# Attention and two MLPs in one kernel: the pooled v through DRAM, the pooled k on VectorE, the root in PSUM, and a new order up to the second tile

## The chip, the cores and the metric

The kernel runs on one core of one Trainium2 chip. The metric is the device time of one execution, in microseconds; it is the median of several runs. Before the change it is 1004.99 us (three runs, 1004.07 to 1005.27).

## The reference

q, k and v are [4, 8, 576, 64] (batch, head, position, channel). The output of the attention is the sum of two attentions, and goes through two MLPs.

```python
q_d, k_d, v_d = [t.reshape(B, H, 144, 4, D).mean(axis=3) for t in (q, k, v)]
out_up = np.repeat(softmax(scale * q_d @ k_d.T) @ v_d, 4, axis=2)      # pooled: 144 x 144 a head
scores = np.where(abs(i - j) < 4, scale * q @ k.T, -1e9)               # local: a band of 7
x = out_up + softmax(scores) @ v                                       # -> [2304, 512]
xn = x / sqrt(mean(x * x, -1) + 1e-6) * rms_g
y = (silu(xn @ w_gate) * (xn @ w_val)) @ w_out                         # 512 -> 1536 -> 512
out = (s * relu(y @ w_in) ** 2 + b) @ w2_out                           # 512 -> 2048 -> 512
```

Both softmaxes subtract the row's maximum and divide by the sum (+ 1e-9). Everything is float32.

## The kernel before

**Tiles.** A row of the MLPs is one position of one batch with its eight heads side by side, 512 channels. A partition holds four neighbouring positions (f = 0 to 3), so a tile is 128 partitions times 4 = 512 rows, and 2304 rows are four whole tiles and one of 256 rows. Tile 0 enters the first MLP in two halves of 256 rows (chunks (0, 1) and (2, 3) of f).

**Pooled attention.** Per batch, four neighbouring rows of q, k and v are summed. q (`pool_q`, L1512) is summed on VectorE in two additions of 128x1152 and 128x576 elements (L1516, L1518); k (`pool_k`, L1127) on GpSimd in three additions of 128x576 (L1133, L1135, L1137). v is needed with 72 partitions, as it is an operand of the last product with the sum over keys in two halves of 72. It is loaded that way (`load_rawv`, L992, two halves a batch into three buffers) and summed in additions of 72x1024 and 72x512: batches 1 and 2 on VectorE (`pool_v`, L1534), batch 3 on GpSimd (`pool_v3`, L1141). Batch 0 has functions of its own (`pool_q0`, `pool_k0`, `pool_v0`) that the change leaves.
TensorE turns the sums (L1835), and for each of 32 heads n computes the scores (L1847), turns the exponentials of head n - 2 (L1858) and multiplies those of head n - 3 with `dv` (L1884). VectorE takes each head's minimum (`least`, L1559), ScalarE its exponentials (`exponents`, L1252) and evacuations (`keep_pooled`, `keep_turned`). `finish_pooled` (L1551) writes `co`, ScalarE stores it to `c_scr` in DRAM (`store_co`), and SyncE loads it back tile by tile as `ct`.

**Local attention.** For each tile, sixteen half heads n: GpSimd multiplies windows of q and k (`qk_mult`, L549, 128x896 elements), VectorE sums (`qk_reduce`, L594); softmax on VectorE and ScalarE (`softmax_max`, `softmax_exp`, `softmax_norm`); then sixteen products of probabilities and windows of v, twelve on GpSimd (`pv_mult`, L563), four on ScalarE (`pv_taps`, L576), again summed on VectorE (L604, L586). The products have two buffers, `prod`, so GpSimd is at most two ahead of VectorE. `add_pooled` adds `ct`, ScalarE sums the squares, VectorE takes the inverse root (`inverse_root`, L673: an estimate from the bits, three Newton steps, each operation on 128x4 elements, each waited for by the next), ScalarE scales (`normalise`), TensorE transposes (L717).

**MLPs.** Numbers are split into a high and a low part and each product is three matrix products. Step s of the first MLP takes 128 of the 1536 hidden columns: `gate` and `val` (L774) with 24 products, `silu` (ScalarE), `hidden_mul` (VectorE, L830), `hidden_hi` (ScalarE), `hidden_lo` (VectorE, L836), and two steps later `out1` (L808 to L810) with 12. Steps 0 to 5 and 6 to 11 are the two halves of tile 0 (256 columns) over the first half of the hidden columns, steps 12 to 17 all of tile 0 (512 columns) over the second; tile 1 begins at step 18. The weights come in 18 pieces through four slots: SyncE loads (`load_piece`, L433), ScalarE makes the high part (`weight_hi`), VectorE or GpSimd the low one (`weight_lo`, L426); a slot is free for the next load once its low part is made.

**Order.** Each engine has its own queue and takes its instructions in the written order; waits are on semaphores and stand in that queue. SyncE issues nearly all loads in a written order, ScalarE the stores. On every engine the order of all this up to the second tile is written out by hand, call by call; later tiles follow tables (`QK_REST`, `PV_LATE` and others). On ScalarE, for one, the end of the second tile's attention stands as follows:

```python
            squares(act, 1, 0)      # L1425
            silu(act, 14)
            pv_taps(act, 1, 13, 0)
            pv_taps(act, 1, 13, 1)
            hidden_hi(act, 14)
            squares(act, 1, 1)
            silu(act, 15)
```

## Time and profile before

| what | value |
|---|---|
| median of the runs | 1004.99 us |
| the profiled execution's own time | 1007.7 us |
| its span, first to last instruction | 1005.6 us |
| TensorE busy | 962.9 us (96%) |
| VectorE, ScalarE, GpSimd busy | 543.8, 354.8, 407.2 us |
| read from and written to HBM | 66.17 and 10.62 MB |

Times in the rows are microseconds from the start of the span of the profiled execution. TensorE is PE, VectorE DVE, ScalarE ACT, GpSimd POOL, SyncE SP. "[a <-b]" behind a row is idle time of the engine before it and the instruction that ended it. An instruction's length includes the time in which it has begun and is held up.

### The profile page before, as it was taken

The numbers are of one execution on the slowest core, as the hardware profiler recorded it, in microseconds if no ns is written. First come the engines' busy times: TensorE is split into PE (matmuls) and PEld (weight loads), VectorE is DVE, ScalarE is ACT, GpSimd is POOL, SyncE is SP. The second block draws the span as 40 slices with busy tenths as digits, with TensorE's granted clock in tenths as the row PEclk, the third lists the DMA queues.
The fourth block names the chain that finished last, engine by engine and source line by source line (L and its number), as shares of the span: only waits on it lengthen the run. The fifth ranks groups of instructions, "written<-read, shape, count | busy, mean of one in ns | idle before, by whom it ended". The sixth has DMA issues, their size and how long they took to land.

```text
span 1005.6 us, 12924 instructions
## 1 busy us (share of the span) xinstructions
PE 962.9 (96%) x4864; PEld 767.7 (76%) x4864; DVE 543.8 (54%) x790; ACT 354.8 (35%) x816; POOL 407.2 (40%) x211
## 2 busy tenths in 40 slices
PE   5899879899999999999999999999999999999997
PEld 4666679766777777777777998888888888888886
...
GB/s 266 227 201 200 110 153 221 119 81 46 141 65 81 39 104 89 27 35 56 38 1 126 85 128 104 42 1 84 1 0 42 42 1 1 64 1 1 0 43 21
DMA packets 53549, 77.62 MB, mean 77 GB/s; under 512 B 6320, under 2 KB 37008, under 8 KB 52464
## 3 DMA queue, kind: packets, MB, share of 16 engines
...
HBM read 66.17 MB, written 10.62 MB: 76 GB/s over the span
## 4 chain that ended last, share of the span: by engine, by line
PE 77%; DVE 5%; POOL 4%; DMA 4%; SPq 3%; ACT 3%; issue 2%; ACTq 0%; DVEq 0%; POOLq 0%
PE bank L774 24%; PE bank L914 7%; PE bank L915 7%; PE bank L916 6%; PE bank L897 6%; PE bank L898 6%; PE bank L896 6%; PE bank L810 4%; PE bank L808 4%; PE bank L809 4%; POOL prod L549 3%; SPq L515 2%; ACT prod_a L576 1%; DMA rawv<-in_v_dram 1%; DMA ks<-in_k_dram 1%
## 5 line engine op out<-in xcount | busy, mean ns | idle before, releaser
L549 POOL TENSOR_TENSOR prod<-qs,ks 128x896 f32<-128x896 f32 x80 | 176.7, 2230 | 90.9 <-DVE sc L594 67.1
L563 POOL TENSOR_TENSOR prod<-sc,vs 128x896 f32<-128x896 f32 x72 | 136.7, 2000 | 47.6 <-DVE x L604 29.0
L935 DVE SCALAR_TENSOR_TENSOR r<-bank,r 128x512 f32<-128x512 f32 (+1 forms) x80 | 51.0, 638 | 181.1 <-ACT r L923 181.1
L898 PE MATMUL bank<-y_h,w2i_l 128*128 128x512 f32 (+1 forms) x320 | 117.7, 368 | 0.0
L923 ACT ACTIVATE r<-bank 128x512 f32<-128x512 f32 (+1 forms) x80 | 44.4, 555 | 182.0 <-PE bank L898 181.3
L830 DVE TENSOR_TENSOR bank<-bank,u 128x512 f32<-128x512 f32 (+1 forms) x66 | 39.5, 599 | 125.4 <-PE bank L774 124.5
L774 PE MATMUL bank<-x_h,wv_h 128*128 128x512 f32 (+1 forms) x264 | 100.9, 393 | 2.6 <-DVE h_l L836 2.6
L808 PE MATMUL bank<-h_h,wo_h 128*128 128x512 f32 (+1 forms) x264 | 103.0, 390 | 0.0
L594 DVE TENSOR_REDUCE sc<-prod 128x14 f32<-128x896 f32 x80 | 85.4, 1077 | 21.4 <-POOL prod L549 21.3
L810 PE MATMUL bank<-h_h,wo_l 128*128 128x512 f32 (+1 forms) x264 | 93.5, 354 | 0.0
L809 PE MATMUL bank<-h_l,wo_h 128*128 128x512 f32 (+1 forms) x264 | 92.8, 351 | 0.0
L774 PE MATMUL bank<-x_h,wg_h 128*128 128x512 f32 (+1 forms) x264 | 89.2, 359 | 2.6 <-ACT u L818 2.5
L774 PE MATMUL bank<-x_l,wv_h 128*128 128x512 f32 (+1 forms) x264 | 91.3, 357 | 0.0
L774 PE MATMUL bank<-x_l,wg_h 128*128 128x512 f32 (+1 forms) x264 | 88.2, 356 | 0.3 <-DVE x_l L752 0.3
L604 DVE TENSOR_REDUCE x<-prod 128x128 f32<-128x896 f32 x72 | 77.6, 1080 | 15.9 <-POOL prod L563 15.3
L914 PE MATMUL bank<-w2o_ha,g_h 128*128 128x512 f32 x216 | 84.3, 390 | 0.4 <-ACT y_st L844 0.4
L915 PE MATMUL bank<-w2o_la,g_h 128*128 128x512 f32 x216 | 84.2, 390 | 0.0
L916 PE MATMUL bank<-w2o_ha,g_l 128*128 128x512 f32 x216 | 84.0, 389 | 0.0
L929 ACT ACTIVATE g_h<-r 128x512 fp32r<-128x512 f32 (+1 forms) x80 | 47.1, 589 | 101.0 <-DVE r L937 101.0
L818 ACT ACTIVATE u<-bank 128x512 f32<-128x512 f32 (+1 forms) x66 | 34.3, 520 | 130.5 <-PE bank L774 129.4
L943 DVE TENSOR_TENSOR g_l<-r,g_h 128x512 fp32r<-128x512 f32 (+1 forms) x80 | 51.1, 639 | 52.5 <-ACT g_h L929 52.5
L824 ACT ACTIVATE h_h<-bank 128x512 fp32r<-128x512 f32 (+1 forms) x66 | 34.2, 519 | 110.7 <-DVE bank L830 110.7
...
## 6 DMA issues: line engine op xcount, KB each, us to landing
...
```

Source lines behind the costliest of these rows:

```text
L549: pool.tensor_tensor(dst, qv, kv, ALU.mult).then_inc(prod_ready, 1)
L563: pool.tensor_tensor(dst, pv, vv, ALU.mult).then_inc(prod_ready, 1)
L594: dve.tensor_reduce(sc[:, a % 2, n * 2 * BAND:(n + 1) * 2 * BAND], prod[:, at_ % 2, :].rearrange("p (s d) -> p s d", d=D), op=ALU.add, axi ...
L604: dve.tensor_reduce(x[:, 2 * half:2 * half + 2, h * D:(h + 1) * D], over(prod[:, at_ % 2, :], [[BAND * D, 2], [BAND, D], [1, BAND]]), op=A ...
L774: last = pe.matmul(o[:, 0:w], wt[:, m, kk, :], xs[:, kk, cols], start=i == 0, stop=i == 3 * DT - 1)
L808: pe.matmul(o, wo_h[:, m, cols], h_h[:, s % 3, 0:w], start=m == 0 and p != 1, stop=False)
L809: pe.matmul(o, wo_h[:, m, cols], h_l[:, s % 3, 0:w], start=False, stop=False)
L810: last = pe.matmul(o, wo_l[:, m, cols], h_h[:, s % 3, 0:w], start=False, stop=m == M1 - 1)
L898: last = pe.matmul(o, w2i_l[:, m, kk, :], y_h[t % 2][:, kk, 0:w], start=False, stop=kk == DT - 1)
L914: pe.matmul(o, g_h[:, r % 3, cols], wh[:, mh, :], start=m == 0, stop=False)
L915: pe.matmul(o, g_h[:, r % 3, cols], wl[:, mh, :], start=False, stop=False)
L916: last = pe.matmul(o, g_l[:, r % 3, cols], wh[:, mh, :], start=False, stop=m == M2 - 1)
```

## The change

- v of batches 1 to 3 is loaded as k and q are, in 128 partitions, but with nine neighbouring rows to a partition, one load a batch, each into a buffer of its own. `pool_v` sums it into `vd` with additions of 128x1152 and 128x576. ScalarE stores `vd` to a DRAM tensor `v_scr` (`store_vd`), and SyncE loads it from there in 72 partitions into `dv` (`load_dv`), waiting for the store and for the buffer. TensorE waits for that load.
- k of batches 1 to 3 is summed by two additions on VectorE, `pool_k(dve, b)`, no longer by three on GpSimd; nor does GpSimd sum v of batch 3.
- The inverse root has its mean, its product and a second copy of its estimate in a PSUM bank: bank 5 (`CTR`) for tile 0, bank 4 (`XT[0]`) for the others. The sums of squares are first brought there by a reduction.
- The low parts of the weights: GpSimd made pieces 0, 1, 2, 5, 7, 9, 11, 13 and 15; it now makes 0, 14 and 17, VectorE the others.
- The order on all queues up to the second tile is written anew.

The diff, with its order lists cut:

```diff
     c_scr = nc.dram_tensor("c_scr", [G, E], F32, kind="Internal").ap()
...
-        rawv += [place([at[0]], "rawv2", [P, H, FAC * D], F32)]
-        at[0] += QT * FAC * D * 4
+        rawv = [None, rawv[1], place(at, "rawv2", [P, QT, FAC * D], F32), rawv[2]]
...
         rawk0_loaded = [sem(f"rawk0_loaded{g}") for g in range(3)]
         rawv0_loaded = [sem(f"rawv0_loaded{g}") for g in range(2)]
         q0_pooled, k0_pooled, v0_pooled = sem("q0_pooled"), sem("k0_pooled"), sem("v0_pooled")
-        rawv_loaded = [sem(f"rawv_loaded{i}") for i in range(3)]
-        q_pooled, k_pooled, v_pooled, k_order = sem("q_pooled"), sem("k_pooled"), sem("v_pooled"), sem("k_order")
-        v3_pooled, v_order = sem("v3_pooled"), sem("v_order")
+        rawv_loaded = [sem(f"rawv_loaded{b}") for b in range(B)]
+        vd_stored, dv_loaded = sem("vd_stored"), [sem("dv_loaded0"), sem("dv_loaded1")]
+        k_order, q_pooled = sem("k_order"), sem("q_pooled")
...
-        def inverse_root(dve, a, c):
-
-            a_link(dve, dve.tensor_scalar(var[:, c], var[:, c] if a else sqs[:, c], 1.0 / E, 1e-6, ALU.mult, ALU.add))
-            dve.tensor_scalar_mul(halfv[:, c], var[:, c], -0.5)
-            a_link(dve, dve.tensor_scalar(rinv[:, c].bitcast(I32), var[:, c].bitcast(I32), -0.5, float(RSQRT_BITS), ALU.mult, ALU.add))
+        def inverse_root(dve, scratch):
+
+            var, newt, root = [scratch[:, i * FAC:(i + 1) * FAC] for i in range(3)]
+            a_link(dve, dve.tensor_scalar(var, var, 1.0 / E, 1e-6, ALU.mult, ALU.add))
+            dve.tensor_scalar_mul(halfv[:, :], var, -0.5)
+            dve.tensor_scalar(rinv[:, :].bitcast(I32), var.bitcast(I32), -0.5, float(RSQRT_BITS), ALU.mult, ALU.add)
+            a_link(dve, dve.tensor_scalar(root.bitcast(I32), var.bitcast(I32), -0.5, float(RSQRT_BITS), ALU.mult, ALU.add))
             for n in range(NEWTON):
-                a_link(dve, dve.tensor_tensor(newt[:, c], rinv[:, c], rinv[:, c], ALU.mult))
-                a_link(dve, dve.tensor_tensor(newt[:, c], newt[:, c], halfv[:, c], ALU.mult))
-                last = dve.scalar_tensor_tensor(out=rinv[:, c], in0=newt[:, c], scalar=1.5, in1=rinv[:, c], op0=ALU.add, op1=ALU.mult)
+                a_link(dve, dve.tensor_tensor(newt, root, rinv[:, :], ALU.mult))
+                a_link(dve, dve.tensor_tensor(newt, newt, halfv[:, :], ALU.mult))
+                if n < NEWTON - 1:
+                    dve.scalar_tensor_tensor(out=root, in0=newt, scalar=1.5, in1=rinv[:, :], op0=ALU.add, op1=ALU.mult)
+                last = dve.scalar_tensor_tensor(out=rinv[:, :], in0=newt, scalar=1.5, in1=rinv[:, :], op0=ALU.add, op1=ALU.mult)
                 if n < NEWTON - 1:
                     a_link(dve, last)
             last.then_inc(rinv_ready, 1)
 
         def inverse_root0(dve):
             dve.wait_ge(sq_ready, FAC)
-            inverse_root(dve, 0, slice(0, FAC))
+            dve.wait_ge(ctr_evac, UNITS * B)
+            a_link(dve, dve.tensor_reduce(CTR[:, 0:FAC], over(sqs[:, 0:], [[1, FAC], [1, 1]]), op=ALU.add, axis=AX.X))
+            inverse_root(dve, CTR)
 
         def inverse_root_of(dve, a):
             dve.wait_ge(sq_ready, 4 + 8 * a)
-            a_link(dve, dve.tensor_tensor(var[:, :], sqs[:, 0:FAC], sqs[:, FAC:2 * FAC], ALU.add))
-            inverse_root(dve, a, slice(0, FAC))
+            a_link(dve, dve.tensor_reduce(XT[0][:, 0:FAC], over(sqs[:, 0:], [[1, FAC], [FAC, 2]]), op=ALU.add, axis=AX.X))
+            inverse_root(dve, XT[0])
+
...
+        def store_vd(eng, b):
+            eng.wait_ge(v_pooled[b], 1)
+            eng.dma_start(v_scr[b].rearrange("(p t) d -> p t d", p=P), vd[:, :, :]).then_inc(vd_stored, 16)
+
+        def load_dv(eng, b):
+
+            eng.wait_ge(vd_stored, 16 * b)
+            wait(eng, cpv, H * (b - 1))
+            eng.dma_start(dv[0:JH, b % 2, :, :], v_scr[b].rearrange("(n p) d -> p n d", p=JH)).then_inc(dv_loaded[b % 2], 16)
...
+        def pool_k(eng, b):
+
+            eng.wait_ge(rawk_loaded[b], 16)
+            rk = rawk[b]
+            eng.tensor_tensor(rk[:, :, 0:2 * D], rk[:, :, 0:2 * D], rk[:, :, 2 * D:4 * D], ALU.add).then_inc(k_half[b], 1)
+            eng.wait_ge(k_half[b], 1)
+            wait(eng, ctr_ps, UNITS * (b - 2) + UNIT.index(("k", 2)) + 1)
+            eng.tensor_tensor(kd[:, b % 2, :, :], rk[:, :, 0:D], rk[:, :, D:2 * D], ALU.add).then_inc(k_pooled[b], 1)
+
+        def pool_v(eng, b):
+
+            eng.wait_ge(rawv_loaded[b], 16)
+            rv = rawv[b]
+            eng.tensor_tensor(rv[:, :, 0:2 * D], rv[:, :, 0:2 * D], rv[:, :, 2 * D:4 * D], ALU.add).then_inc(v_half[b], 1)
+            eng.wait_ge(v_half[b], 1)
+            wait(eng, vd_stored, 16 * (b - 1))
+            eng.tensor_tensor(vd[:, :, :], rv[:, :, 0:D], rv[:, :, D:2 * D], ALU.add).then_inc(v_pooled[b], 1)
 
         @block.sync
...
 
             def load_rawv0(g):
-                sp.dma_start(rawv0[0:JH, H * g:H * (g + 1), :], v_rows[0][:, H * g:H * (g + 1), :]).then_inc(rawv0_loaded[g], 16)
-
-            def load_rawv(b, g):
-
-                i = 2 * (b - 1) + g
-                wait(sp, v_pooled, i - 2)
-                sp.dma_start(rawv[i % 3][0:JH, :, :], v_rows[b][:, H * g:H * (g + 1), :]).then_inc(rawv_loaded[i % 3], 16)
+                sp.dma_start(rawv0[0:JH, H * g:H * (g + 1), :], v0_rows[:, H * g:H * (g + 1), :]).then_inc(rawv0_loaded[g], 16)
+
+            def load_rawv(b):
+                sp.dma_start(rawv[b][:, :, :], v_rows[b]).then_inc(rawv_loaded[b], 16)
...
-            load_rawv0(0)
             sp.wait_ge(consts_made, 3)
             load_qk(sp, 0, 0)
+            load_rawv0(0)
...
             load_qk(sp, 0, 1)
+            load_qk(sp, 0, 2)
+            load_rawv0(1)
             load_rawk(1)
-            load_rawv0(1)
-            load_qk(sp, 0, 2)
-            load_rawv(1, 0)
+            load_qk(sp, 0, 3)
+            load_rawv(1)
             load_qk(sp, 0, 4)
-            load_rawv(1, 1)
-            load_qk(sp, 0, 3)
+            load_qk(sp, 0, 5)
             load_rawq(2)
+            load_dv(sp, 1)
             load_rawk(2)
-            load_qk(sp, 0, 5)
-            load_rawv(2, 0)
-            load_v(sp, 0, 0)
-            load_qk(sp, 0, 7)
             load_qk(sp, 0, 6)
             with nc.allow_non_contiguous_dma(reason="512 gains, one a partition and slice"):
                 sp.dma_start(gcol[:, :], rms_g.rearrange("(k p) -> p k", p=P)).then_inc(small_loaded, 16)
             sp.dma_start(sbcol[:, 0:1], s2.partition_broadcast(P)).then_inc(small_loaded, 16)
             sp.dma_start(sbcol[:, 1:2], b2.partition_broadcast(P)).then_inc(small_loaded, 16)
-            load_rawv(3, 0)
+            load_qk(sp, 0, 7)
+            load_rawv(2)
+            load_v(sp, 0, 0)
+            load_v(sp, 0, 3)
+            load_v(sp, 0, 1)
             load_rawq(3)
+            load_dv(sp, 2)
+            load_v(sp, 0, 2)
             load_rawk(3)
-            load_piece(sp, 0)
...
             load_v(sp, 0, 6)
+            load_v(sp, 0, 7)
+            load_piece(sp, 0)
+            load_ct(sp, 0)
+            load_dv(sp, 3)
+            load_qk(sp, 1, 0)
...
             qk_mult(pool, 0, 2)
             qk_mult(pool, 0, 3)
-            pool_k(1)
             qk_mult(pool, 0, 4)
...
             qk_mult(pool, 0, 9)
-            pool_k(2)
             qk_mult(pool, 0, 10)
...
             qk_mult(pool, 0, 15)
-            pool_v3(0)
-            pool_k(3)
             pv_mult(pool, 0, 0)
...
             pv_mult(pool, 0, 12)
             pv_mult(pool, 0, 14)
-            weight_lo(pool, 1)
             pv_mult(pool, 0, 15)
             qk_mult(pool, 1, 0)
+            qk_mult(pool, 1, 1)
             weight_lo(pool, 0)
-            pool_v3(1)
-            qk_mult(pool, 1, 1)
             qk_mult(pool, 1, 2)
-            weight_lo(pool, 2)
             qk_mult(pool, 1, 3)
             qk_mult(pool, 1, 4)
             qk_mult(pool, 1, 5)
-            weight_lo(pool, 5)
             qk_mult(pool, 1, 6)
...
             pv_mult(pool, 1, 15)
+            weight_lo(pool, 14)
+            weight_lo(pool, 17)
...
             exponents(8)
+            store_vd(act, 1)
...
+            store_co(act, 0)
+            store_vd(act, 2)
             keep_turned(14)
...
-            pv_taps(act, 0, 6, 1)
+            store_vd(act, 3)
             exponents(24)
...
@@ -1422,16 +1420,19 @@
             pv_taps(act, 1, 10, 0)
             pv_taps(act, 1, 10, 1)
             hidden_hi(act, 13)
+            pv_taps(act, 1, 13, 0)
+            silu(act, 14)
+            pv_taps(act, 1, 13, 1)
             squares(act, 1, 0)
-            silu(act, 14)
-            pv_taps(act, 1, 13, 0)
-            pv_taps(act, 1, 13, 1)
             hidden_hi(act, 14)
+            weight_hi(act, 15)
+            weight_hi(act, 16)
+            silu(act, 15)
+            weight_hi(act, 17)
             squares(act, 1, 1)
-            silu(act, 15)
+            normalise(act, range(FAC), 2)
             hidden_hi(act, 15)
             silu(act, 16)
-            normalise(act, range(FAC), 2)
             hidden_hi(act, 16)
             split_hi(act, 2, 0)
             split_bf(act, 2, 0)
...
-            def pool_v(b, g):
-
-                i = 2 * (b - 1) + g
-                rv = rawv[i % 3][0:JH, :, :]
-                dve.wait_ge(rawv_loaded[i % 3], 16 * (i // 3 + 1))
-                c_link(dve.tensor_tensor(rv[:, :, 0:2 * D], rv[:, :, 0:2 * D], rv[:, :, 2 * D:4 * D], ALU.add))
-                if b >= 2:
-                    dve.wait_ge(cpv, H * (b - 2) + 4 * g + 4)
-                dve.tensor_tensor(dv[0:JH, b % 2, H * g:H * (g + 1), :], rv[:, :, 0:D], rv[:, :, D:2 * D], ALU.add).then_inc(v_pooled, 1)
...
+            qk_reduce(dve, 0, 4)
             least(7)
-            pool_v(1, 0)
-            qk_reduce(dve, 0, 4)
+            pool_k(dve, 1)
             qk_reduce(dve, 0, 5)
             least(8)
-            exponent_sums(0, 1)
-            pool_v(1, 1)
             qk_reduce(dve, 0, 6)
+            pool_v(dve, 1)
+            qk_reduce(dve, 0, 7)
+            finish_pooled(0, 0)
             least(9)
-            least(10)
...
-            pv_reduce(dve, 0, 7)
-            finish_pooled(2, 0)
+            pool_v(dve, 3)
             least(24)
-            pv_reduce(dve, 0, 8)
-            pv_reduce_act(dve, 0, 6)
+            pv_reduce_act(dve, 0, 10)
             pv_reduce(dve, 0, 9)
+            pv_reduce(dve, 0, 11)
             least(25)
             exponent_sums(2, 1)
-            pv_reduce(dve, 0, 11)
-            pv_reduce_act(dve, 0, 10)
...
             pv_reduce(dve, 0, 15)
             add_pooled0(dve, 1)
-            qk_reduce(dve, 1, 0)
-            least(28)
+            weight_lo(dve, 1)
             least(29)
             inverse_root0(dve)
             least(30)
+            qk_reduce(dve, 1, 0)
             exponent_sums(3, 0)
             finish_pooled(2, 1)
-            weight_lo(dve, 3)
             least(31)
             qk_reduce(dve, 1, 1)
             exponent_sums(3, 1)
+            qk_reduce(dve, 1, 2)
             dve.wait_ge(small_loaded, 48)
             split_lo(dve, 0, 0)
             split_lo(dve, 0, 1)
-            qk_reduce(dve, 1, 2)
             qk_reduce(dve, 1, 3)
+            weight_lo(dve, 3)
+            weight_lo(dve, 2)
             weight_lo(dve, 4)
             hidden_mul(dve, 0)
+            finish_pooled(3, 0)
+            hidden_lo(dve, 0)
             qk_reduce(dve, 1, 4)
...
+            qk_reduce(dve, 1, 15)
             hidden_mul(dve, 7)
-            qk_reduce(dve, 1, 14)
+            qk_reduce(dve, 2, 0)
             hidden_lo(dve, 7)
             hidden_mul(dve, 8)
-            qk_reduce(dve, 1, 15)
+            softmax_max(dve, 1)
             hidden_lo(dve, 8)
-            softmax_max(dve, 1)
+            weight_lo(dve, 9)
+            weight_lo(dve, 10)
+            qk_reduce(dve, 2, 1)
+            softmax_norm(dve, 1)
             hidden_mul(dve, 9)
-            weight_lo(dve, 14)
-            qk_reduce(dve, 2, 0)
-            softmax_norm(dve, 1)
             hidden_lo(dve, 9)
+            pv_reduce(dve, 1, 0)
             hidden_mul(dve, 10)
...
-                        if b == 0:
-                            pe.wait_ge(v0_pooled, h // 4 + 1)
-                        elif b < B - 1:
-                            pe.wait_ge(v_pooled, 2 * (b - 1) + h // 4 + 1)
-                        else:
-                            pe.wait_ge(v3_pooled, h // 4 + 1)
-                    if h == 0:
+                    if b == 0 and h % 4 == 0:
+                        pe.wait_ge(v0_pooled, h // 4 + 1)
+                    if b and h == 0:
+                        pe.wait_ge(dv_loaded[b % 2], 16 * ((b + 1) // 2))
                         wait(pe, co_ready, 2 * b - 1)
                     if h == 4:
                         wait(pe, co_ready, 2 * b)
```

## Rows read from the trace of the kernel before

**Rows 1.** The page, section 1: busy time of each engine.

```profile
PE 962.9 (96%) x4864; PEld 767.7 (76%) x4864; DVE 543.8 (54%) x790; ACT 354.8 (35%) x816; POOL 407.2 (40%) x211
```

**Rows 2.** Busy by stretch: PE, PEld, DVE, ACT, POOL (instructions), clock, DMA share, GB/s.

```profile
14.40:118.60 104.20, 89.74 (x490) 67.84 (x489) 90.68 (x107) 57.97 (x226) 86.72 (x42) 1.00 0.84 203
...
138.30:190.50 52.20, 49.29 (x396) 46.30 (x394) 42.19 (x55) 28.12 (x46) 49.39 (x21) 1.00 0.65 200
360.00:1005.00 645.00, 639.90 (x3131) 519.04 (x3128) 273.74 (x444) 190.15 (x347) 132.54 (x64) 1.00 0.13 42
```

**Rows 3.** TensorE's waits from 138 us on (us, times, longest); two stretches as above.

```profile
PE bank L774 <- DVE h_l L836: 2.6, 1, 2.6
PE bank L774 <- ACT u L818: 2.5, 2, 2.2
...
190.00:195.00 5.00, 4.50 (x25) 4.22 (x26) 4.55 (x8) 4.18 (x17) 4.81 (x3) 0.66 0.04 8
225.00:235.00 10.00, 7.76 (x28) 4.74 (x27) 6.86 (x20) 5.74 (x15) 2.45 (x2) 0.83 0.17 45
```

**Rows 4.** TensorE in order of time: start, length, line, operation, [idle before].

```profile
131.86 1.94 PE L717 MATMUL bank<-ident,x 128*128 128x128 f32 x8 [7.12 <-ACT x L698]
...
138.32 1.20 PE L774 MATMUL bank<-x_h,wg_h 128*128 128x256 f32 x4
...
248.32 1.52 PE L774 MATMUL bank<-x_h,wg_h 128*128 128x512 f32 x4
```

**Rows 5.** VectorE in order of time, the inverse root of tile 0.

```profile
118.89 2.19 DVE L676 TENSOR_SCALAR halfv<-var 128x4 f32<-128x4 f32 x1
...
121.19 7.59 DVE L679 TENSOR_TENSOR newt<-rinv 128x4 f32<-128x4 f32 x1
...
130.19 0.16 DVE L681 SCALAR_TENSOR_TENSOR rinv<-newt,rinv 128x4 f32<-128x4 f32 x1
```

**Rows 6.** GpSimd in order of time beside it.

```profile
121.13 1.27 POOL L1149 TENSOR_TENSOR dv<-rawv 72x512 f32<-72x512 f32 x1
...
126.42 2.34 POOL L426 TENSOR_TENSOR wg_l<-raww,wg_h 128x1024 bf16<-128x1024 f32 x1
```

**Rows 7.** Lines of VectorE up to 250 us: min/median/max ns; last: one instruction.

```profile
L830 DVE TENSOR_TENSOR bank<-bank,u x18: 414/422/700, 143.6 to 244.5; 128x256 f32<-128x256 f32 x12, 128x512 f32<-128x512 f32 x6
...
L1542 DVE TENSOR_TENSOR dv<-rawv x4: 686/1384/2447, 38.4 to 87.7; 72x512 f32<-72x512 f32 x4
...
L1516 DVE TENSOR_TENSOR rawq<-rawq x3: 1341/1343/1929, 20.5 to 74.3; 128x1152 f32<-128x1152 f32 x3
...
3.85 0.30 DVE L1509 TENSOR_TENSOR mask<-mask,band_t 128x140 f32<-128x140 f32 x1
```

**Rows 8.** VectorE by lines, 14.4 to 118.6 us: busy, mean, idle before.

```profile
L594 DVE TENSOR_REDUCE sc<-prod 128x14 f32<-128x896 f32 x17 | 18.1, 1074 | 3.5 <-POOL prod L549 3.4
...
L1539 DVE TENSOR_TENSOR rawv<-rawv 72x1024 f32<-72x1024 f32 x4 | 8.5, 2118 | 3.6 <-DMA rawv<-in_v_dram 3.6
L1518 DVE TENSOR_TENSOR qd<-rawq 128x576 f32<-128x576 f32 x3 | 7.8, 2607 | 0.1
L1542 DVE TENSOR_TENSOR dv<-rawv 72x512 f32<-72x512 f32 x4 | 5.9, 1475 | 0.1
L1516 DVE TENSOR_TENSOR rawq<-rawq 128x1152 f32<-128x1152 f32 x3 | 4.6, 1538 | 0.0
```

**Rows 9.** GpSimd by lines, the same stretch.

```profile
L549 POOL TENSOR_TENSOR prod<-qs,ks 128x896 f32<-128x896 f32 x17 | 38.7, 2293 | 15.6 <-DMA ks<-in_k_dram 13.9 <-DVE sc L594 1.7
...
L1137 POOL TENSOR_TENSOR kd<-kd,rawk 128x576 f32<-128x576 f32 x3 | 5.1, 1696 | 0.2
```

**Rows 10.** The tensor c_scr: landing time of its transfers.

```profile
DMA to landing us min/median/max: 2.6/3.1/4.8
```

**Rows 11.** VectorE by lines and forms, 138.3 to 190.5 us.

```profile
L594 DVE TENSOR_REDUCE sc<-prod 128x14 f32<-128x896 f32 x15 | 16.0, 1077 | 5.2 <-POOL prod L549 5.2
L426 DVE TENSOR_TENSOR wv_l<-raww,wv_h 128x1024 bf16<-128x1024 f32 x3 | 6.5, 2180 | 1.4 <-ACT wv_h L412 1.4
```

288 lines of the change are left out of this document (130 added, 158 removed).

## The prediction

> **What bounds the kernel now.** I read the page first. TensorE is busy for 963 of 1005.6 us [rows 1], so whatever the change does must either start its dense work earlier or close gaps in it. The table by stages says where those gaps are: from 360 us on TensorE is busy for 639.9 of 645.0 us, while from 14.4 to 118.6 us it has 89.7 of 104.2, and from 138.3 to 190.5 us 49.3 of 52.2 [rows 2]. After the first dense matrix product at 138.32 us TensorE waits for another engine five times or so, 6.6 us in all, 2.6 for VectorE's `h_l` and 2.5 for ScalarE's `u` being most of it; these two are followed by a granted clock of 0.66 over 5 us and of 0.83 over 10 us [rows 3]. So the end moves with two quantities: T, the start of that first product (138.3 us), and S, the stretch from there to the first product of tile 1 at 248.3 us, thus 110.0 us. What follows S is full, and the change leaves its instructions as they are.
>
> What sets T: TensorE's own queue is through with head 31's scores and the turning of head 29 at 124.74 us, then stands 7.12 us for x of tile 0, and from the transposes at 131.86 us it needs 6.46 us to T [rows 4]. x waits for the inverse root on VectorE, about 118.7 to 130.35 us: twelve instructions on four elements, ten of them about 0.16 us long, but one 2.19 and one 7.59 us [rows 5]. Beside it GpSimd runs without a break: the 7.59 us begin as `dv<-rawv` begins (121.13), and end as `wg_l` ends (128.76) [rows 6]. The root therefore holds 9.5 us in which VectorE stands behind GpSimd.
>
> **The root in PSUM.** Each of its operations now has an operand in bank 5 (tile 0) or 4. The nearest rows with such an operand don't stretch: 414 to 422 ns for half and more of the products into the bank (the 700 is the doubled width), while the same engine's addition `dv<-rawv`, all operands in SBUF, goes from 686 to 2447 ns for one shape [rows 7]. The new root has 16 instructions, since it sums first and writes the estimate twice. From 128.8 to 130.35 us the last eight ran in 1.6 us, 0.2 us each [rows 5], so 16 are 3.2 us; I take 3.5. The bounds are 3.2 and, if the bank doesn't help, the old 11.7 us. Gain on the path: 8.2 us. The roots of tiles 1 to 4 are three instructions longer, 0.6 us each, hidden behind TensorE's full steps.
> The Trainium skill (VectorE: DVE Perf Modes, "The TRN2 errata — SBUF-src ops pay a fixed extra latency per instruction") speaks against this step: its table gives VectorE 120 cycles of fixed cost with a PSUM source against 58 for SBUF, so an estimate from that page is 16 times 65 ns, 1.0 us more. The trace shows no such difference: 422 ns for 256 elements from the bank and 300 ns for 140 from SBUF leave about 0.15 us of fixed cost each at one element a cycle [rows 7].
>
> **The sums on VectorE.** Before the root VectorE was busy 90.7 of 104.2 us [rows 2]. The change takes away four pairs of v sums of 72 partitions (8.5 + 5.9 = 14.4 us) and moves one reduction of tile 1 (1.07 us) behind the root [rows 8]. It adds three pairs for k and three for v, each a 128x1152 and a 128x576 addition like those of q: 4.6 + 7.8 us for three pairs, 4.1 us a pair, 24.8 us for six [rows 8]; and one weight subtraction, 1.2 us, since it has no more elements than the 128x1152 one. Bounds of a pair: 2.0 us if neither waits for GpSimd (1.34 + 0.69), 6.6 if it stands behind two products of 2.3 us, all that the two buffers of `prod` allow [rows 7, 9]. I take the q rows, as they are the same shapes in the same stage. Busy time becomes 90.7 - 15.5 + 26.0 = 101.2 us.
> Idle time was 13.5 us, 3.6 of it for rawv by DMA and 3.5 for GpSimd's products [rows 8], the rest for scores, for ScalarE's taps and for `co`. GpSimd loses three k sums of three additions, some 1.6 us each, 14 us, and also 6 us of v3 and one subtraction of 2.3 before its last tile-0 product [rows 6, 9], so its part goes; v comes as one load in more partitions. I leave 5 us of idle time (bounds 0 and 13.5). The root then starts at 14.4 + 101.2 + 5 = 120.6 us instead of 118.7, and ends at 124.1 instead of 130.35: 6.2 us earlier. TensorE's own queue is released by the minima on the same engine and comes at 124.74 + 1.9 = 126.6, later than x (124.1 and one scaling of two rows, 1.3 us). So the queue ends the wait, not the root: transposes at 126.7, T = 133.2 us, **5.1 us earlier**. What is late next is VectorE's order of minima.
>
> **v through DRAM.** Each batch adds a store of 0.29 MB on ScalarE's queue and a load of as much, in pieces of 256 bytes, on SyncE's. The same kind of way exists: from issue to landing of a transfer of `c_scr` are 2.6 to 4.8 us, in the middle 3.1 [rows 10]. So 5 to 10 us for the two, and up to 12 with the queues' own waits, from the sum to TensorE. Batches 1 and 2 have room: batch 2's sum ends well over 10 us ahead of head 16. SyncE's wait for the store of batch 1 holds back everything behind it, rawk2 and the windows of heads 6 and 7 among them; by the durations above VectorE is through with batch 1's v sum 33 us into the stretch, so the wait falls at about 48 to 55 us. Head 6's first product is reduced thirteenth, which by the same count comes at 65 us. The held loads, some 2.4 MB at the 203 GB/s of this stretch [rows 2], take 12 us up to then. I cost this at nothing; without the cover of VectorE's load it is up to 5 us. Batch 3 has little room: between its sum and the minimum of head 27, next to which TensorE needs it, stand three more minima, five reductions of 1.07 us [rows 8] and 1.0 us of small work, in all 7.8 us, against 5 to 12 us. Nothing where I take 7, 4 us at the other end.
>
> **S, 110.0 us.** Subtractions of weights go from GpSimd to VectorE: from 138.3 to 190.5 us VectorE had six, 12.7 us (three of them in the row shown, 2.18 each), and was busy 42.2 of 52.2 us [rows 2, 11]; it now has nine there, 6.3 us more, 48.5 of 52: it still fits. ScalarE loses nothing. The 2.6 us gap at 190.5 us stands behind the softmax and a subtraction; in the new order two subtractions, a reduction and the whole softmax lie between the products of steps 8 and 9, so I keep this gap and its clock loss. The gap before 227.6 us (2.2 us of the 2.5) came from ScalarE held in the squares of tile 1 until GpSimd's products were summed. GpSimd loses six subtractions of 2.4 us and more and v3's second half in this part, and the order puts silu(15) ahead of the squares: this gap goes, and with it the clock loss, 0.17 x 10 = 1.7 us [rows 3]. I charge 1.0 us for the fuller VectorE. S becomes 110.0 - 2.2 - 1.7 + 1.0 = 107.1 us, **2.9 us less**. Weights 14 and 17 now wait for the end of tile 1's products on GpSimd; step 16 needs 14 at about T + 87 = 220 us, and GpSimd, some 20 us lighter, is through before that.
>
> **Sum.** 5.1 + 2.9 = 8.0 us. The profiled execution took 1007.7 us (span 1005.6); it becomes 999.7. The runs' median, 1004.99, lies 2.7 us below it, so the median of the new kernel is **997.0 us**.
>
> **The rivals.**
> A. *VectorE's sums hardly wait.* GpSimd has 22 us less to do in 100, so it stands idle oftener. With 2.0 us a pair the six cost 12.2 instead of 24.8 us, and T could come 12 us earlier still; TensorE's 14.5 us of idle time in the stretch [rows 2] would allow some 8 of these. Time 989. For it: two of the three 128x1152 additions took 1.34 us [rows 7]. Against it: the three 128x576 ones took 2.6 us in the mean [rows 8].
> The Trainium skill (SBUF — State Buffer, "Who interferes with whom") says that an addition with two SBUF inputs contends with a GpSimd instruction that reads SBUF, and that the loser waits for the whole of one instruction. The 7.59 us behind four instructions that follow each other almost without a gap [rows 5, 6] are longer than that rule allows; the 128x576 rows fit it. By the rule a pair waits for two instructions at most, an estimate that is the upper bound above and changes no term.
> B. *Batch 3 comes late from DRAM* or SyncE's wait leaves the windows late. Decided if store, wait and load take over 8 us. TensorE is then 3 to 4 us later: T 137, gain 1.3 + 2.9, time 1001.
> C. *The root still waits* although it has a PSUM operand; the change then doesn't do what it says, and VectorE's added load stays. Root from 120.6 to 132.3, T = 140.3, S - 2.9: 1004.1 us, no change.
> D. *Slower: VectorE becomes the bound of S.* Its nine subtractions at 2.9 us instead of 2.2 make 48.5 into 55 of 52 us; every gap then costs as the known one, 2.6 us and 1.7 us of clock [rows 3]. Two more such gaps take the gain, the third decides: 997.0 + 3 x 4.3 = 1009.9. For it: VectorE carries the products and remainders on which TensorE waits, behind those subtractions. Against: tile 1's reductions hardly wait for GpSimd any more, which were 5.2 us of idle time there [rows 11].
>
> **How the numbers follow.** Forecast 0.48 (own range 992 to 1002), A 0.14, B 0.12, C 0.10, D 0.16. Faster or slower by over 0.2% (2 us) is about what can be told from no change. Faster: forecast, A, B, 0.74; same: C, 0.10; slower: D, 0.16. The range reaches into A and up to the edge of D: 987 to 1008.
>
> **What would show it.** The root's instructions all near 0.2 us, against C. The start of the root at 120 us and q, k and v additions at 4 us a pair; at 2 us a pair A is right. The first 256-wide product at 133 us. A wait of TensorE's `dv,cpT` products for a DMA in heads 24 to 27 is B. TensorE waits of over 2 us between T and T + 107 beyond one are D. From there on the two traces should run side by side, 8 us apart. The prediction is wrong if T moves by less than 2 us, or if a gap opens after tile 1 has begun.

## The result, and the profile after

The changed kernel takes **991.12 us** (median of four runs, 990.15 to 995.06) against 1004.94; the ratio is 0.9871, interval 0.9843 to 0.9899. The forecast was 997.0 with 987 to 1008: right in sign and inside the range, 5.9 us too high. The profiled executions differ by more than the medians, 988.6 against 1005.6 us of span, 17.0 us. That of the kernel before took 1007.7 us, 2.8 more than its median, and it was late ahead of the root: b_plus_root below, the same program up to there, began its root at 115.48 us, this one at 118.69.

The page, section 1 [rows 1]: GpSimd lost 33 us, VectorE gained 3, TensorE lost 4.

```profile
PE 958.5 (97%) x4864; PEld 765.3 (77%) x4864; DVE 546.6 (55%) x816; ACT 355.4 (36%) x816; POOL 373.7 (38%) x192
```

Busy time by stretch, columns as in [rows 2]: the pooling stage, the 52 us behind T, and the end of S.

```profile
14.40:118.60 104.20, 94.11 (x524) 72.49 (x522) 97.65 (x129) 60.80 (x236) 70.80 (x31) 1.00 0.79 224
...
125.39:177.60 52.21, 51.36 (x423) 48.79 (x422) 45.51 (x62) 27.46 (x55) 35.58 (x16) 1.00 0.55 155
...
220.00:231.20 11.20, 9.18 (x40) 6.10 (x38) 7.62 (x10) 5.30 (x9) 9.40 (x5) 0.85 0.29 80
```

TensorE in order of time, beside [rows 4]: the last scores of its own queue, the transposes, T, and the first product of tile 1.

```profile
116.70 0.69 PE L1857 MATMUL bank<-ident,cs 72*72 72x72 f32 x4
118.94 1.94 PE L724 MATMUL bank<-ident,x 128*128 128x128 f32 x8 [1.54 <-ACT x L705]
...
125.39 1.20 PE L779 MATMUL bank<-x_h,wg_h 128*128 128x256 f32 x4
...
231.22 1.52 PE L779 MATMUL bank<-x_h,wg_h 128*128 128x512 f32 x4
```

T came from 138.32 to 125.39, 12.9 us earlier; S fell from 110.0 to 105.83, 4.2 us less; behind it the kernels take 757.4 and 757.3 us (988.6 - 231.2, 1005.6 - 248.3). So the whole gain lies ahead of tile 1, as forecast, and three quarters of it in T. Of the 12.9 us of T, 9.0 lie between the start of the root and T (19.6 us before, 10.6 after), and 3.9 ahead of the root, where the execution of before was late by most of that.

The root of tile 0 on VectorE, beside [rows 5]: its first instruction, the two kinds that waited before, and its last. All 16 take 0.15 to 0.17 us, 2.64 us in all from 114.78, with GpSimd at work beside it up to 116.7.

```profile
114.78 0.15 DVE L693 TENSOR_REDUCE bank<-sqs 128x4 f32<-128x4 f32 x1
...
115.16 0.16 DVE L677 TENSOR_SCALAR halfv<-bank 128x4 f32<-128x4 f32 x1
...
115.51 0.17 DVE L681 TENSOR_TENSOR bank<-bank,rinv 128x4 f32<-128x4 f32 x1
...
117.26 0.16 DVE L685 SCALAR_TENSOR_TENSOR rinv<-bank,rinv 128x4 f32<-128x4 f32 x1
```

VectorE by lines, 14.4 to 118.6 us, beside [rows 8]: busy, mean, idle before. These are the three pairs of q, k and v, and the subtraction that joined them.

```profile
L995 DVE TENSOR_TENSOR kd<-rawk 128x576 f32<-128x576 f32 x3 | 7.2, 2392 | 0.1
L1004 DVE TENSOR_TENSOR vd<-rawv 128x576 f32<-128x576 f32 x3 | 7.2, 2392 | 0.1
L1519 DVE TENSOR_TENSOR qd<-rawq 128x576 f32<-128x576 f32 x3 | 5.4, 1805 | 0.1
L1517 DVE TENSOR_TENSOR rawq<-rawq 128x1152 f32<-128x1152 f32 x3 | 4.6, 1520 | 0.3 <-DMA rawq<-in_q_dram 0.3
L1001 DVE TENSOR_TENSOR rawv<-rawv 128x1152 f32<-128x1152 f32 x3 | 4.0, 1349 | 0.0
L992 DVE TENSOR_TENSOR rawk<-rawk 128x1152 f32<-128x1152 f32 x3 | 4.0, 1341 | 0.0
...
L426 DVE TENSOR_TENSOR wv_l<-raww,wv_h 128x1024 bf16<-128x1024 f32 x1 | 3.1, 3103 | 0.0
```

Waits from T to tile 1 on TensorE (us, times, longest), beside [rows 3], and SyncE's wait in its queue for the stores of v:

```profile
PE bank L724 <- DVE x_l L757: 2.8, 2, 1.9
PE bank L724 <- ACT x L705: 1.3, 1, 1.3
...
SPq L982 <- DMA v_scr<-vd: 36.1, 3, 18.1
```

The waits for `h_l` and `u` of 2.6 and 2.2 us are gone. Of those left 0.85 us stand at 149.29, and the kernel before had that one too (0.8); the other 3.3 us, 1.31 for x and 1.95 for `x_l`, stand at the first transposes of tile 1, with the clock loss of the row of 220 us above (0.85). SyncE waited 36 us, and TensorE never for `dv` of the batches 1 to 3.

### The profile page after: what moved, and what is told of

The parts are those of the page before. It is cut to its first block, busy times and chain, and to the rows that moved or that the text cites. A ratio compares the mean times of both kernels' runs of the same rounds, so it can differ in the third digit from the quotient of the medians.

```text
span 988.6 us, 12936 instructions
## 1 busy us (share of the span) xinstructions
PE 958.5 (97%) x4864; PEld 765.3 (77%) x4864; DVE 546.6 (55%) x816; ACT 355.4 (36%) x816; POOL 373.7 (38%) x192
## 3 DMA queue, kind: packets, MB, share of 16 engines
q1 hardware_dynamic: 52444, 71.79, 24.7%
## 4 chain that ended last, share of the span: by engine, by line
PE 81%; DVE 8%; DMA 3%; ACT 3%; issue 2%; POOL 2%; SPq 1%; ACTq 0%; DVEq 0%; POOLq 0%
PE bank L779 24%; PE bank L919 7%; PE bank L920 7%; PE bank L921 7%; PE bank L903 7%; PE bank L901 7%; PE bank L902 7%; PE bank L815 4%; PE bank L813 4%; PE bank L814 4%; PE bank L1846 2%; DMA ks<-in_k_dram 2%; POOL prod L549 1%; PE bank L1879 1%; DVE x L604 1%
## 5 line engine op out<-in xcount | busy, mean ns | idle before, releaser
L549 POOL TENSOR_TENSOR prod<-qs,ks 128x896 f32<-128x896 f32 x80 | 181.3, 2288 | 91.2 <-DVE sc L594 71.0
L815 PE MATMUL bank<-h_h,wo_l 128*128 128x512 f32 (+1 forms) x264 | 93.2, 353 | 0.0
```

The lines of the kernel that those rows point to most:

```text
L549: pool.tensor_tensor(dst, qv, kv, ALU.mult).then_inc(prod_ready, 1)
L815: last = pe.matmul(o, wo_l[:, m, cols], h_h[:, s % 3, 0:w], start=False, stop=m == M1 - 1)
```

## The experiments

In this table T is the first 256-wide product, R the first instruction of the inverse root of tile 0, tile 1 the first product of tile 1, all of the profiled execution. E is the start of VectorE's 128x576 addition of q of batch 1, some 21 us in: it depends on the first loads alone. R - E leaves out how late the first loads came, but not what later transfers add; T - R is the stretch in which the two roots differ. The ratios go by the runs of the kernel before that were taken beside each.

| kernel | median us (range) | ratio to before | E | R | T | R - E | T - R | tile 1 |
|---|---|---|---|---|---|---|---|---|
| before | 1004.9 |  | 21.88 | 118.69 | 138.32 | 96.8 | 19.6 | 248.32 |
| after | 991.1 (990.2-995.1) | 0.987 | 21.59 | 114.78 | 125.39 | 93.2 | 10.6 | 231.22 |
| b_plus_root | 999.3 (996.2-1004.1) | 0.9956 [0.9933, 0.998] | 21.63 | 115.48 | 130.30 | 93.9 | 14.8 | 239.25 |
| b_plus_k | 1010.5 (1005.9-1013.6) | 1.0045 [1.0019, 1.007] | 23.31 | 122.89 | 143.02 | 99.6 | 20.1 | 252.33 |
| b_plus_root_k | 1005.6 (1002.7-1010.6) | 1.0013 [0.9992, 1.0034] | 22.85 | 120.81 | 135.63 | 98.0 | 14.8 | 243.75 |
| a_minus_root | 995.4 (993.5-998.4) | 0.9904 [0.9874, 0.9934] | 22.28 | 115.84 | 127.81 | 93.6 | 12.0 | 235.99 |
| a_minus_k | 1004.2 (999.3-1010.3) | 0.9993 [0.9965, 1.002] | 20.91 | 125.68 | 136.31 | 104.8 | 10.6 | 242.63 |
| a_minus_root_k | 1009.1 (1005.1-1014.2) | 1.0042 [1.0019, 1.0066] | 24.65 | 134.48 | 146.43 | 109.8 | 12.0 | 254.48 |
| a_direct | 989.6 (988.2-991.5) | 0.9846 [0.9822, 0.987] | 21.47 | 114.08 | 124.70 | 92.6 | 10.6 | 231.32 |
| a_direct_minus_k | 994.6 (992.6-997.3) | 0.9894 [0.9871, 0.9917] | 21.61 | 117.87 | 128.49 | 96.3 | 10.6 | 234.80 |
| a_double_v | 993.4 (993.2-996.9) | 0.9892 [0.9867, 0.9916] | 21.04 | 116.59 | 127.21 | 95.6 | 10.6 | 233.08 |
| a_improved | 990.3 (988.1-992.4) | 0.9847 [0.9809, 0.9885] | 21.50 | 112.19 | 123.70 | 90.7 | 11.5 | 230.16 |
| a_weights_pool | 991.5 (990.9-991.6) | 0.986 [0.9845, 0.9874] | 23.31 | 114.71 | 124.69 | 91.4 | 10.0 | 232.45 |
| a_root1_first | 992.2 (990.7-993.3) | 0.9867 [0.9849, 0.9885] | 24.99 | 118.17 | 128.79 | 93.2 | 10.6 | 234.04 |

Kernels that are the same program up to R show how far R - E can be trusted. Before and b_plus_root have 96.8 and 93.9 us, and part at waits for loads of v and for `c_scr` (at 29, 59 and 72 us); b_plus_k and b_plus_root_k have 99.6 and 98.0, a_minus_k and a_minus_root_k 104.8 and 109.8; after, a_minus_root and a_root1_first lie within 0.4. So the root is read from T - R, and a difference in R - E below 3 us is read beside the medians.

### The root alone, put in and taken back

b_plus_root is the kernel before with the new root and nothing else:

```diff
-            inverse_root(dve, 0, slice(0, FAC))
+            a_link(dve, dve.tensor_reduce(CTR[:, 0:FAC], over(sqs[:, 0:], [[1, FAC], [1, 1]]), op=ALU.add, axis=AX.X))
+            inverse_root(dve, CTR)
```

> The kernel before with one part of the change, the inverse root in a PSUM bank; all orders and sums stay. T is the start of the first 256-wide matrix product (before 138.3 us), S the way from there to the first product of tile 1 (110.0). Theory (the root stood behind GpSimd's unbroken run): its instructions are all near 0.17 us, it ends near 121.5 us, TensorE's own queue at 124.7 sets the transposes, T = 131.3; GpSimd's wait of 5.6 us for the reduction behind the root goes too, so S stays at 110: time 998. Rival 1 (the gain is given back in S, where GpSimd's subtractions and products set tile 1): T = 131.3 but S = 114 to 117, time 1002 to 1005. Rival 2 (a PSUM operand is no help): T and time as before.

999.31 us. T came 8.0 us earlier, but 3.2 of these were won before the root began:

```profile
115.48 0.17 DVE L693 TENSOR_REDUCE bank<-sqs 128x4 f32<-128x4 f32 x1
```

The root took 2.6 us in place of 11.7, and T - R fell by 4.8 us, from 19.6 to 14.8; with k on VectorE it falls by 5.3 (20.1 to 14.8). The medians say the same, 4.7 and 4.9 us. GpSimd's instructions beside it are the same as in [rows 6]. The wait did not vanish from VectorE, it went to the next instruction with both inputs in SBUF:

```profile
119.62 7.04 DVE L426 TENSOR_TENSOR wv_l<-raww,wv_h 128x1024 bf16<-128x1024 f32 x1
```

TensorE's transposes started at 121.33 with no wait, and they did not need that subtraction. But the minimum of head 31 stands behind it on VectorE (126.58 us), and TensorE then waited for that head's exponentials:

```profile
127.94 0.69 PE L1865 MATMUL bank<-ident,cs 72*72 72x72 f32 x4 [2.33 <-ACT cs L1265]
```

So 2.3 us of what the root gave were paid back ahead of T. a_minus_root is the changed kernel with the old root.

> The changed kernel with its inverse root back in SBUF, as in the kernel before; everything else stays. T was 125.4 us. Theory (a VectorE addition waits only while GpSimd's instructions follow one another without a gap; here GpSimd finishes wg_l at 116.7 and then waits for a reduction that stands behind the root): one stall of about 1.8 us, less four instructions of 0.2, T = 126.4, time +1, 992. Rival (the root in SBUF costs what it did in the kernel before, 8 to 9 us): T = 134, time 1000.

995.35 us, 4.2 more than after. Here one instruction waits, not for 7.6 us but for 1.9:

```profile
115.84 1.94 DVE L677 TENSOR_SCALAR var<-sqs 128x4 f32<-128x4 f32 x1
...
119.67 0.16 DVE L683 SCALAR_TENSOR_TENSOR rinv<-newt,rinv 128x4 f32<-128x4 f32 x1
```

It follows that a bank as operand does keep the root clear of GpSimd; and that in the new order, where GpSimd has one instruction beside the root (`wg_l` to 117.8) and not four in a row, the old root takes 1.4 us more, not 9. T - R is 12.0 against 10.6 there, and 19.6 against 14.8 in the kernel before; the median's 4.2 has 2.3 us of S in it. So the rest of the change, with the old root, brings T - R from 19.6 to 12.0 us, and the bank brings a further 1.4. As a_minus_root_k below has 12.0 too, with k on GpSimd, it is the order around the root (or the new v) that wins most of T.

### k on VectorE, taken back and put in

a_minus_k gives the sums of k of batches 1 to 3 back to GpSimd, three additions each, in the places that they had:

```diff
-            pool_k(dve, 1)
...
+            qk_mult(pool, 0, 3)
+            pool_kp(1)
```

> The changed kernel with k of batches 1 to 3 summed on GpSimd again, three additions each, after its 4th, 10th and 16th product. Theory (VectorE's load sets T, and it stands still only while GpSimd works): VectorE loses 11 us of k sums, but GpSimd is 14 us busier before tile 0's last product, and stalls of the v, q and softmax instructions come back, some 7 us; its products come later too. T within 3 us of 125.4, time 989 to 994. Rival 1 (VectorE's busy time alone counts): T = 118 to 120, time 985. Rival 2 (GpSimd's own queue sets T once it sums k): T = 131 or more, time 997.

1004.24 us: the whole gain is gone. The second rival held, that GpSimd's queue then sets T, but for the most part not because of its work. GpSimd by lines, 14.4 to 118.6 us:

```profile
L1164 POOL TENSOR_TENSOR kd<-rawk 128x576 f32<-128x576 f32 x3 | 4.2, 1396 | 24.7 <-DMA rawk<-in_k_dram 24.7
```

A sum takes 4.2 us, three additions of 1.4, and not the 7 that the expectation of b_plus_k puts down (21 us for three); what costs is the 24.7 us in which GpSimd stands ahead of it with its products behind. rawk is late since SyncE issues it behind its wait for the store of v of the batch before. b_plus_k and b_plus_root_k do the opposite, k on VectorE in the kernel before, without and with the new root.

> The kernel before with the sums of k of batches 1 to 3 on VectorE in two additions each, at the places of the kernel after (ahead of its sums of v); root in SBUF, v in 72 partitions, all orders else as before. Theory: GpSimd loses 21 us of work and VectorE gains 3 x 3.7 = 11 us, of which its 13.5 us of idle time ahead of the root take most; the root starts 117 to 121, and GpSimd, that much earlier, no longer has several products in a row beside it, so the root takes 3 to 5 us instead of 11.7: T 130 to 133, 996 to 1000 us. Rival: with SyncE's old order k comes late and VectorE waits for it, or the additions stand in the port behind GpSimd: root starts 124 or later and keeps its long wait, T 138 or more, 1004 to 1009 us.

> The same with the root in PSUM as well. Theory: root 2.6 us, beginning 117 to 121; TensorE's own queue then sets T (it was 130.3 with the root alone, and nothing of the pooling branch held it): T 129 to 130, 997 to 999 us, no better than the root alone (999.3). Rival, the two parts of the change carry it all: 991 to 994 us as the kernel after, T 125 to 126, since the long waits of TensorE for k and q ahead of T shrink as well.

1010.5 and 1005.6 us: b_plus_k did what its rival said and a little more, b_plus_root_k came out above both of its ranges. By the medians k on VectorE costs 5 to 6 us with either root. VectorE by lines in b_plus_k, same stretch:

```profile
L1511 DVE TENSOR_TENSOR kd<-rawk 128x576 f32<-128x576 f32 x3 | 7.2, 2387 | 0.1
...
L1509 DVE TENSOR_TENSOR rawk<-rawk 128x1152 f32<-128x1152 f32 x3 | 6.7, 2237 | 0.0
L1535 DVE TENSOR_TENSOR dv<-rawv 72x512 f32<-72x512 f32 x4 | 5.9, 1479 | 0.1
...
L1532 DVE TENSOR_TENSOR rawv<-rawv 72x1024 f32<-72x1024 f32 x4 | 5.4, 1343 | 0.0
```

k adds 13.9 us, while v in 72 partitions still takes 11.3 us for two batches; in the changed kernel 11.2 us do all three. And the long wait is there again (7.58 us at 125.89), as GpSimd has its four instructions in a row. So the parts do not add up: k on VectorE is a loss of 5 us alone and a gain of 13 in the changed kernel. Most of that gain goes back to SyncE's wait (below). Why it is a loss alone is shown in part: up to R VectorE was as busy in b_plus_root_k as in the changed kernel (89.3 and 88.7 us), but idle 8.6 against 4.5 us, 3.2 of it for ScalarE's taps and 1.4 for `c_scr`, waits that the changed kernel does not have. The room that v in 128 partitions leaves on VectorE cannot be much of it by these times, 11.3 us against 11.2; no run takes the new v alone.

> The kernel after with both taken back: the root works in SBUF again and the sums of k of batches 1 to 3 are GpSimd's again. Alone, the first cost 4.2 us (995.35 against 991.12) and the second 13.1 (1004.24). Theory: with k on GpSimd its queue sets T (the first 256-wide product, 136.31 there), and the root, 2.6 us long, had room ahead of that; a root that waits for the port 2 to 9 us longer is partly covered: T 136 to 140, 1004 to 1008 us. Rival: the costs add (991.1 + 4.2 + 13.1 = 1008.4) because GpSimd, fuller again, holds the root as long as in the kernel before (9 us, one instruction of 7.6): T 142 to 145, 1008 to 1013 us, slower than the kernel before.

a_minus_root_k has the new v, its way through DRAM and all new orders, with the old root and k on GpSimd: 1009.12 us, slower than before. The medians add, as the rival said, but not by its mechanism: the root waited 1.94 us, as in a_minus_root, and T - R is 12.0, as there. What is more lies ahead of the root, where the program is that of a_minus_k: R - E is 109.8 against 104.8 us, and GpSimd's wait for rawk grew from 24.7 to 29.7. The profiled execution is the slowest of the ten (1014.2, median 1009.1). The two kernels with the store's wait and k on GpSimd scatter over 11 and 9 us in ten runs each, a_direct_minus_k without that wait over 5 in four: the chain of store, wait and load may add to lateness, which was not tried.

### SyncE's wait

a_direct takes the wait for the store away by loading `dv` from every fourth row of v; a_direct_minus_k does that to a_minus_k. Both leave out the sum of v for the last product, so they compute something else and serve as a measurement only; VectorE still makes and stores the sums, and ScalarE waits for the stores once, behind the root, when they have long landed.

```diff
-            eng.wait_ge(vd_stored, 16 * b)
-            eng.dma_start(dv[0:JH, b % 2, :, :], v_scr[b].rearrange("(n p) d -> p n d", p=JH)).then_inc(dv_loaded[b % 2], 16)
+            eng.dma_start(dv[0:JH, b % 2, :, :], v[b].rearrange("h (n p f) d -> p (h n) f d", n=2, f=FAC)[:, :, 0, :]).then_inc(dv_loaded[b % 2], 16)
```

> The kernel after, in which v of the batches 1 to 3 for the values is loaded straight from the input (every fourth row of v), with no wait for the store of the sums; VectorE still makes and stores the sums, but the values are made of the unsummed rows. It takes away only SyncE's waits for the store (about 36 us in all, at most 18 at one) and what stands behind them in its queue (rawk2, the pieces behind dv of batch 2, ct and heads behind dv of batch 3). Theory: those waits cost nothing, as TensorE never waited for dv or for k of batches 2 and 3: T 125.4, 990 to 992 us. Rival: SyncE's waits delayed the heads for GpSimd's products, whose lateness shows as VectorE's idle time; T 122 to 124, 987 to 989 us.

> The kernel after with the sums of k of batches 1 to 3 on GpSimd (as in a_minus_k, 1004.24 us, T 136.31), and with v of batches 1 to 3 for the values loaded straight from every fourth row of v (as in a_direct), so that SyncE's queue has no wait for a store; the values are made of unsummed rows. It asks why k on GpSimd cost 13 us. Theory 1, GpSimd stood in its queue for rawk (24.7 us of its idle time there), which SyncE issued late behind its wait for the store: without that wait GpSimd doesn't wait, T 126 to 130, 992 to 996 us. Theory 2, it is GpSimd's work itself, 3 sums of about 7 us (21 us) in a queue that had some 33 us of room ahead of T, and the wait for rawk is only where that room went: then T stays at 134 to 137, 1001 to 1005 us. Between them, both count about half: T 131 to 133.

989.58 and 994.56 us. In the changed kernel the wait costs 0.6 us of R - E and 1.5 of the median, too little to tell from nothing. With k on GpSimd it costs 8.5 us (R - E 104.8 against 96.3; 9.7 by the medians): theory 1. What k on GpSimd costs beside that is 3.7 us (96.3 against 92.6; 5.0 by the medians); in it are 14.2 us of additions and 7.1 us in which GpSimd still stands for rawk, and no run parts the two. SyncE's queue around it, in a_minus_k and then in a_direct_minus_k:

```profile
48.18 0.32 SPq L982 DMA_DIRECT2D dv<-v_scr  x1
48.54 0.65 SPq L1021 DMA_DIRECT2D rawk<-in_k_dram  x1
```

```profile
29.45 5.74 SPq L983 DMA_DIRECT2D dv<-in_v_dram  x1
35.23 5.88 SPq L1022 DMA_DIRECT2D rawk<-in_k_dram  x1
```

rawk of batch 2 leaves 13 us later behind the wait. The load from every fourth row is itself slow to issue, 5.7 us against 0.3.

### What VectorE's time is worth, and the order ahead of the roots

a_double_v makes the second addition of v twice.

> The kernel after in which the second addition of v of each of the batches 1 to 3 (128x576, 2.5 us waiting, about 0.8 us otherwise) is made twice, with the same operands: 3 instructions, 7.5 us more on VectorE, all of it ahead of the root of tile 0. Theory, VectorE's queue sets T in the kernel after (busy 94.2 of 100.4 us before the root): its 6.2 us of idle time are waits for TensorE or for data that another delay can use up in part only; root 4 to 7 us later, T 129 to 132.5, 995 to 998 us. Rival, there is room, since TensorE's own queue sets T and the root ended 1.5 us before it mattered: T 125.4 to 127, 991 to 993 us.

993.39 us. The repeated additions never waited for GpSimd, though the first ones always did, so they were 2.3 us and not 7.5:

```profile
L1004 DVE TENSOR_TENSOR vd<-rawv 128x576 f32<-128x576 f32 x3 | 7.2, 2389 | 0.1
...
L1006 DVE TENSOR_TENSOR vd<-rawv 128x576 f32<-128x576 f32 x3 | 2.3, 757 | 0.1
```

R - E rose by 2.4 us for these 2.3, T - R not at all, and the median by 2.3; VectorE's idle time up to R stayed (4.5 and 4.6 us). So in the changed kernel a microsecond on VectorE ahead of the root was a microsecond of the kernel. The time lies beside the rival's 991 to 993 and not in the theory's 995 to 998: my number was wrong with the size of the load, and it is the unchanged idle time and T - R that speak for the theory.

Three orders tried to use that. a_improved puts the subtraction of piece 1 behind root 0, and those of pieces 15 and 16 behind root 1; a_weights_pool gives the three to GpSimd; a_root1_first moves only 15 and 16:

```diff
+            inverse_root_of(dve, 1)
             weight_lo(dve, 15)
             weight_lo(dve, 16)
-            inverse_root_of(dve, 1)
```

> The changed kernel with two subtractions of weights on VectorE moved behind the inverse root of their tile: piece 1 behind the root of tile 0 and the minimum of head 30, pieces 15 and 16 behind the root of tile 1. In the changed kernel piece 1 took 3.1 us just ahead of the root and TensorE then stood 1.5 us for x; pieces 15 and 16 took 6.5 us ahead of tile 1's root and TensorE stood 1.3 and 1.9 us for x and its low part. Theory: T = 123.9 (TensorE's own queue sets it), S shorter by 1.3 to 3, time 986.5 to 988.5. Rival (other work on the same queue is next, x_l and the products behind them): no change, 991.

> The kernel after with three subtractions of weights, pieces 1, 15 and 16 (3.1, 3.4 and 3.1 us on VectorE), on GpSimd, right behind its pieces 0 and 14. Theory: piece 1 is off the way to the first root without a debt behind it, so T falls by 1.5 us as in a_improved (123.70) and no wait for piece 1 takes its place; the root of tile 1 starts 6 us earlier and the waits for x and x_l of 3.2 us around it go: T 123.5 to 124.5, tile 1 at 226 to 228, 986 to 988 us. Rival: GpSimd's products behind the pieces come 3 to 7 us later, VectorE and then TensorE wait for them (h_l, u), and nothing is won: 990 to 993 us.

> The kernel after with one change of VectorE's order: the root of tile 1 ahead of the two subtractions of pieces 15 and 16 (3.43 and 3.12 us beside GpSimd), not behind them. Theory: T stays at 125.4; in the kernel after TensorE waits 1.3 us for x and 2.8 for x_l around the first transposes of tile 1 and loses its full clock for some 6 us with them, and in a_improved, with the same order there, only 0.8 us for x_l was left; the first product of tile 1 at 228 (S 102.5), 987 to 989 us, 2 to 3 us less than the kernel after and a little less than a_improved. Rival: pieces 15 and 16, or the h_l behind them, are what TensorE then waits for, and the gain stays below 1 us: 230 or later, 990 to 991.5 us.

990.27, 991.45 and 992.17 us: none is told apart from after. What each took away came back as the wait for the next thing: 2.9 us for the moved `wv_l` in a_improved, 4.7 us for `u` in a_weights_pool, where ScalarE stood 4.5 us for a load of weights ahead of it, and in a_root1_first again the moved piece:

```profile
PE bank L779 <- DVE wv_l L426: 2.6, 1, 2.6
PE bank L724 <- ACT x L705: 1.5, 1, 1.5
PE bank L724 <- DVE x_l L757: 1.5, 2, 0.8
```

The wait for x in these lines is the one ahead of T (1.54 us in after). At tile 1 stand 2.6 us for `wv_l` and 0.8 for `x_l`, in place of the 3.3 us for x and `x_l`. Its S is 105.25 against 105.83.

a_root1_first also shows what a single execution can tell. Up to T it is the same program as after, instruction for instruction, yet its T is 3.4 us later. The q addition and T of after, and then of a_root1_first:

```profile
21.59 0.76 DVE L1519 TENSOR_TENSOR qd<-rawq 128x576 f32<-128x576 f32 x1
...
125.39 1.20 PE L779 MATMUL bank<-x_h,wg_h 128*128 128x256 f32 x4
```

```profile
24.99 0.76 DVE L1519 TENSOR_TENSOR qd<-rawq 128x576 f32<-128x576 f32 x1
...
128.79 1.20 PE L779 MATMUL bank<-x_h,wg_h 128*128 128x256 f32 x4
```

The difference is 3.40 us at 21 us and 3.40 us at T. In this pair the first loads alone set it, and then the schedule ran stiffly. It does not always: before and b_plus_root were 0.25 us apart at E and 3.2 at R.

## Why the prediction was right, and where it was off

**What bounds the kernel** held: the end moved with T and S, and with nothing else.

**The root in PSUM** held: 16 instructions in 2.64 us, 3.5 forecast, no wait (rival C falls). What it is worth on the path was put at 8.2 us; in the kernel before it was 4.8, in the new order 1.4. The estimate from the Trainium skill's table (VectorE: DVE Perf Modes, "The TRN2 errata — SBUF-src ops pay a fixed extra latency per instruction") made it 1.0 us dearer with a PSUM source. The trace has 0.15 to 0.17 us for these instructions from the bank and 0.16 us for those from SBUF, so here there is no such difference.

**The start of the root** was the first miss: 120.6 forecast, 114.8 measured. Idle time came as said (6.2, 5 forecast); busy time was 94.2 and not 101.2 us. Six pairs of k and v took 22.4 us, not 24.8, since no 128x1152 addition waited; those of q 10.0, not 12.4; v of batch 0 6.0, not 7.8; three instructions of the softmax took 0.39 us each, where two had taken 1.45 and 1.05 us beside GpSimd. I left these last three groups at their old durations, though the same step took 22 us off the engine that held them. Against that the one subtraction cost 3.1 us, not 1.2: it waited as an SBUF instruction does. The start was counted on from 118.69 us, in an execution that was late: the same program in b_plus_root began its root at 115.48, so VectorE's part of the change gained hardly anything ahead of the root. It took k off GpSimd at no cost.

**TensorE's own queue** was the second miss. I let it follow the root's start by the same 6.0 us as before, hence 126.6. The sentence that the minima on VectorE release that queue was the step that failed. In the kernel before TensorE had stood 3.6 us for ScalarE, and 0.3 us more for the next copy of the same kind, and was late from there on:

```profile
115.67 1.22 PE L1884 MATMUL bank<-dv,cpT 72*72 72x64 f32 x8 [3.58 <-ACT cpT L1250]
```

The copy `cpT` of head 25 stood in ScalarE's order behind the last taps, two squares of tile 0 and a piece of weights; the new order puts it ahead of the squares and the weights. In the changed kernel TensorE did not wait once from 94.4 us to the end of its own queue at 117.4, 2.6 us behind the root's start. So x ended the wait again, at 118.94. Against the forecast 133.2: 5.8 us from the start of the root and 2.0 from the queue. The list of ScalarE's order held this, and I had not followed it.

**v through DRAM** held for TensorE: the stores landed 2.1 to 2.8 us after their issue, SyncE then issued the loads, and the wait for `dv` of batches 1 to 3 never came (rival B falls); the trace has no landing time for the loads. The sentence "I cost this at nothing" holds only with the cover that it names: with k on GpSimd the same wait of SyncE cost 8.5 us.

**S**: 107.1 forecast, 105.83 measured, by two errors. The gap at the softmax, which I kept, was gone with its clock loss (51.36 of 52.21 us busy, clock 1.00). No run asks why. In its place came waits of 3.3 us at tile 1's first transposes, behind two subtractions of 3.4 and 3.1 us ahead of root 1. After them the granted clock was 0.85 over 11 us, the lower of the two levels (1.2 GHz) for part of it. That is rival D's mechanism once, where it needed three.

**The number** was right by its range, and right in saying where the gain would end. The sum made the gain 8.0 us; the medians moved by 13.8. In the traces T's 5.1 us were 12.9, some 3 of them the lateness of one execution, and S's 2.9 were 4.2. What was too small is the stretch from the root to T: the working had it 8.2 us shorter by the root and lost much of that to TensorE's queue, where the order had made room.

**Rival A** came nearest to the number (989) with a wrong reason: the pairs took 3.7 us, not 2.0. Its other half came out, that T could fall 8 us below the forecast: TensorE's idle time from 14.4 us to T went from 21.9 to 10.4 us.
